# Attention's value product with the values as weights, in high and low halves for nine of sixteen pairs, written straight into the dense stage's input

## The chip, the cores and the metric

The kernel runs on one core of a Trainium2 chip. The metric is the device time of one execution in microseconds (us), of which the median of several runs is quoted. Lower is better.

## What is computed

```python
def _attn_ref(q, k, v, tau):                      # 4 batches, 8 heads, 576 rows, head size 64
    scores = scale * np.matmul(q, k.transpose(0, 1, 3, 2))
    thresh = np.max(scores, axis=-1, keepdims=True) - tau
    scores = np.where(scores >= thresh, scores, -1000000000.0)
    scores = scores - np.max(scores, axis=-1, keepdims=True)
    attn = np.exp(scores)
    attn = attn / (np.sum(attn, axis=-1, keepdims=True) + 1e-09)
    return np.matmul(attn, v)
...
    xk = mu_k * x + (1.0 - mu_k) * x_prev         # first dense stage, x is 4 x 576 x 512
    xr = mu_r * x + (1.0 - mu_r) * x_prev
    k = np.maximum(xk @ w_k, 0.0)
    v = k * k @ w_v
    r = 1.0 / (1.0 + np.exp(-(xr @ w_r)))
    x = r * v
...
    u = x + np.real(np.fft.fft(np.fft.fft(x, axis=1), axis=2))
    un = (u - mean) / np.sqrt(var + 1e-06)        # over the 512 channels
    return u + np.maximum(un @ w_ch1, 0.0) @ w_ch2
```

## The kernel before

**Numbers.** float32 data go through the matrix engine in one of two ways. "Native" is a matmul on float32 operands, which the program emits as two instructions. "In halves" is fp32r: a value is split into a high part (rounded to fp32r) and a low part (the rest), and a product is the sum of fp32r matmuls high x high, low x high and high x low (`three`, lines 706 to 709).

**Work and its order.** Heads are taken in pairs: 16 pairs, four to a batch. A pair has 9 row tiles of 128 queries: tiles 0 to 3 of the first head, tile 4 with the last 64 rows of both heads, tiles 5 to 8 of the second. There are 144 tiles. Every engine runs a loop over slots n (lines 919 to 926 on PE). In slot n:

- PE forms the scores of tile n (`qk`, line 734), transposes the probabilities of tile n-3 (`transpose_probs`, line 747: five blocks of 128 keys), multiplies the transposed probabilities of tile n-4, as weights, with the 64 columns of values (`pv`, line 764, native), and then does its share of the dense work of the batch before.
- DVE takes the row maximum of tile n (`row_max`, line 1235), masks and sums tile n-1 (`mask`, line 1249), and does its share of the dense work.
- ACT forms exp of tile n (line 985), does its share of the dense work, and copies the transposed probabilities of tile n-2 out of PSUM in two pieces (`copy_units`, line 994). At the end of a head `copy_head` (line 1007) copies the head's output into x_att, scaled by the reciprocal row sums.
- POOL splits q and k of the next heads (lines 548 and 556) and forms low halves for the dense stage.
- SP issues the loads.

Each engine works in its own program order. From tile 36 on one PSUM buffer holds scores, so that `qk(n)` waits for `row_max(n-1)`.

**Dense work beside it.** A batch's dense stage runs beside the attention of the next one, at phases counted in slots from the batch's last tile plus one. X_AT (2 to 5): PE transposes x_att (`dense`, lines 839 and 844) and DVE and ACT copy it into xT. MIX_AT (3 to 20): ACT, DVE, ACT and POOL form the mixed inputs mix_v, mix_h and mix_l. Phases 8 to 35: the groups r, k and v, 12 matmuls of 288 columns for a group of r or k and 24 for one of v. FOLD_AT (32, 35): sums on DVE for the Fourier transform. Y_AT (36 to 38) and U_AT (39 to 43): its matmuls, then the additions on POOL (`add_dft`, line 638). So phases 36 to 43 of one batch fall on the first pair of the batch after the next one's start, together with phases 0 to 7 of the next batch. The last batch's dense stage runs alone, and the closing two-layer stage (`mlp`) follows it.

```python
MIX_AT = [3, 4, 5, 6, 7, 8, 9, 10, 12, 13, 14, 15, 17, 18, 19, 20]
U_AT = [39, 39, 42, 42, 43]
...
last = nc.tensor.matmul(bank(6 + p)[:, i * DH:i * DH + width], probsT[:, n % 2, kt * P128:(kt + 1) * P128],
                        v_sb[:, kt, pair % 2, p * DH:p * DH + width], start=kt == 0, stop=kt == KT - 1)
```

## Time and profile before

| | |
|---|---|
| median of 3 runs | 1123.1 us (1122.18 to 1124.58) |
| the profiled execution | 1122.31 us |
| its span in the trace | 1120.5 us |
| PE busy | 1080.2 us, 96% |
| DVE, ACT, POOL busy | 559.9, 515.5, 420.0 us |
| row maxima, first and last start | 9.3 and 578.7 us |

The span is that of the instructions; the rest of the execution lies around it. Busy shares are means over stages with different limits. A matmul's printed duration holds its way through the array, so that matmuls in a row overlap: what one costs is the distance from its start to the next start. The stretches below were cut where the first row maximum of a pair starts: pair 0 starts at 9.3, pair 4 (batch 1) at 93.4, pair 8 at 245.9, pair 12 at 415.5, pair 13 at 459.1, pair 14 at 498.7, pair 15 at 541.7; the last tile's row maximum starts at 578.7.

### The profile page before, as it was taken

The numbers are of one execution on the slowest core, as the hardware profiler recorded it, in microseconds if no ns is written. First come the engines' busy times: TensorE is split into PE (matmuls) and PEld (weight loads), VectorE is DVE, ScalarE is ACT, GpSimd is POOL, SyncE is SP. The second block draws the span as 40 slices with busy tenths as digits, with TensorE's granted clock in tenths as the row PEclk, the third lists the DMA queues.
The fourth block names the chain that finished last, engine by engine and source line by source line (L and its number), as shares of the span: only waits on it lengthen the run. The fifth ranks groups of instructions, "written<-read, shape, count | busy, mean of one in ns | idle before, by whom it ended". The sixth has DMA issues, their size and how long they took to land.

```text
span 1120.5 us, 19690 instructions
## 1 busy us (share of the span) xinstructions
PE 1080.2 (96%) x7476; PEld 1055.1 (94%) x7476; DVE 559.9 (50%) x1109; ACT 515.5 (46%) x1269; POOL 420.0 (37%) x367
## 2 busy tenths in 40 slices
PE   6999999999999999899998998999999999999998
PEld 6899999998899998899996997999999999999998
DVE  7998764576464575564552557453132321323211
ACT  5989775656666646775653733221111111111110
POOL 5897652543662543652512363431111121110100
PEclk9999999999899999999997998999999999999999
DMA  9544101141301141301112107301001010010000
GB/s 244 167 115 151 56 24 34 49 132 35 97 24 34 38 141 36 98 24 34 40 65 94 43 10 281 118 1 57 1 1 57 1 56 0 0 56 0 29 1 29
DMA packets 38353, 69.26 MB, mean 62 GB/s; under 512 B 4214, under 2 KB 19708, under 8 KB 37244
## 3 DMA queue, kind: packets, MB, share of 16 engines
q1 hardware_dynamic: 37964, 67.80, 19.2%
q8 instruction: 53, 0.87, 0.3%
q10 hardware_dynamic: 304, 0.33, 0.1%
q14 instruction: 32, 0.26, 0.1%
HBM read 55.84 MB, written 12.28 MB: 61 GB/s over the span
## 4 chain that ended last, share of the span: by engine, by line
PE 82%; DVE 5%; POOL 5%; issue 3%; ACT 3%; DMA 0%; SPq 0%; DVEq 0%; POOLq 0%; ACTq 0%
PE PB L707 21%; PE PB L709 19%; PE PB L708 19%; PE PB L764 10%; PE PB L734 6%; PE PB L747 5%; DVE probs L1249 1%; POOL mix_l L607 1%; DVE neg_s L1235 1%; POOL q_hl L556 1%; POOL x2T L638 1%; POOL k_lo L548 1%; POOL fold_l L630 1%; ACT exps L985 1%; POOL x2T L639 1%
## 5 line engine op out<-in xcount | busy, mean ns | idle before, releaser
L1187 ACT ACTIVATE h_hi<-PB 128x384 fp32r<-128x384 f32 x96 | 47.2, 492 | 334.7 <-PE PB L709 334.7
L1416 DVE SCALAR_TENSOR_TENSOR h_lo<-PB,h_hi 128x384 fp32r<-128x384 f32 x96 | 53.5, 557 | 260.7 <-ACT h_hi L1187 260.7
L764 PE MATMUL PB<-v_sb,probsT 128*128 128x64 f32 (+1 forms) x1440 | 179.3, 272 | 0.0
L764 PEld LDWEIGHTS PB<-v_sb,probsT 128*128 128x128 f32 x1440 | 174.1, 194 | 0.0
L994 ACT ACTIVATE probsT<-PB 128x384 f32<-128x384 f32 (+1 forms) x288 | 109.3, 432 | 81.6 <-PE PB L747 80.5
L1249 DVE SCALAR_TENSOR_TENSOR probs<-neg_s,thresh,exps 128x576 f32<-128x576 f32 x144 | 145.8, 1012 | 0.0
L1235 DVE TENSOR_SCALAR_CACHE_REDUCE neg_s<-PB,taus 128x576 f32<-128x576 f32 x144 | 117.1, 813 | 40.4 <-PE PB L734 35.8
L707 PE MATMUL PB<-un_h,w1h 128*128 128x384 f32 x384 | 132.3, 345 | 0.0
L709 PE MATMUL PB<-h_hi,w2l 128*128 128x384 f32 x384 | 129.4, 337 | 0.0
L707 PE MATMUL PB<-h_hi,w2h 128*128 128x384 f32 x384 | 129.3, 337 | 0.0
L708 PE MATMUL PB<-un_l,w1h 128*128 128x384 f32 x384 | 129.2, 337 | 0.0
L708 PE MATMUL PB<-h_lo,w2h 128*128 128x384 f32 x384 | 129.2, 336 | 0.0
L709 PE MATMUL PB<-un_h,w1l 128*128 128x384 f32 x384 | 129.1, 336 | 0.0
L985 ACT ACTIVATE exps<-neg_s,negmax 128x576 f32<-128x576 f32 x144 | 111.0, 771 | 0.0
L607 POOL TENSOR_TENSOR mix_l<-mix_v,mix_h 128x288 fp32r<-128x288 f32 x64 | 53.4, 834 | 150.8 <-ACT mix_h L1070 119.9
L747 PE MATMUL PB<-ident,probs 128*128 128x128 f32 x720 | 103.2, 274 | 5.2 <-ACT probsT L994 4.3
L747 PEld LDWEIGHTS PB<-ident,probs 128*128 128x128 f32 x720 | 86.1, 141 | 7.0 <-issue 6.1
L734 PE MATMUL PB<-k_hi,q_hl 128*128 128x288 f32 x320 | 74.7, 315 | 10.0 <-DVE q_hl L1220 7.6
L622 POOL TENSOR_TENSOR k_sql<-k_sq,k_sqh 128x288 fp32r<-128x288 f32 x56 | 48.5, 870 | 90.9 <-DVE k_sq L1331 90.8
L1268 DVE SCALAR_TENSOR_TENSOR mix_v<-xT,mus,mix_v 128x288 f32<-128x288 f32 x64 | 45.7, 713 | 70.8 <-ACT mix_v L1056 70.4
L707 PE MATMUL PB<-mix_h,wkh 128*128 128x288 f32 x256 | 78.8, 308 | 0.9 <-POOL mix_l L607 0.8
L707 PE MATMUL PB<-k_sqh,wvh 128*128 128x288 f32 x256 | 78.7, 307 | 0.1
(154 smaller groups left out, 2485.8 us busy)
## 6 DMA issues: line engine op xcount, KB each, us to landing
q_raw<-qT_dram SPq DMA_DIRECT2D x62, 160.0 KB, 3.1
k_raw<-kT_dram SPq DMA_DIRECT2D x64, 144.0 KB, 3.1
w_raw<-w_dram SPq DMA_DIRECT2D x8, 1024.0 KB, 9.4
cs<-cs_scr SPq DMA_DIRECT2D x4, 1740.0 KB, 7.8
u_scr<-x2T SPq DMA_DIRECT2D x4, 1152.0 KB, 5.2
u_in<-u_scr SPq DMA_DIRECT2D x6, 768.0 KB, 5.0
out_dram<-o_sb SPq DMA_DIRECT2D x24, 192.0 KB, 1.9
cd<-cd_scr SPq DMA_DIRECT2D x4, 1032.0 KB
```

The costliest lines, as they stand in the source:

```text
L607: nc.gpsimd.tensor_tensor(mix_l[kind][:, dt, :], mix_v[:, i % 2, :], mix_h[kind][:, dt, :].bitcast(F32), ALU.subtract).then_inc(mixl_ready, 1)
L707: nc.tensor.matmul(o, ah, rh, start=start, stop=False)
L708: nc.tensor.matmul(o, ah, rl, start=False, stop=False)
L709: return nc.tensor.matmul(o, al, rh, start=False, stop=stop)
L734: last = nc.tensor.matmul(scores(n)[:, half, :], q_hl[:, h, i * P128:(i + 1) * P128], kk[:, h, half * HALF:half * HALF + HALF], start=h == ...
L747: last = nc.tensor.transpose(bank(4 + unit % 2)[:, (kt - k0) * P128:(kt - k0 + 1) * P128], probs[:, n % 2, kt * P128:(kt + 1) * P128], ide ...
L764: last = nc.tensor.matmul(bank(6 + p)[:, i * DH:i * DH + width], probsT[:, n % 2, kt * P128:(kt + 1) * P128], v_sb[:, kt, pair % 2, p * DH ...
L985: nc.scalar.activation(exps[:, n % 2, :], neg_s[:, n % 2, :], ACT.Exp, bias=negmax[:, col:col + 1], scale=-1.0).then_inc(exp_ready, 1)
L994: nc.scalar.activation(probsT[:, n % 2, k0 * P128:k1 * P128], bank(4 + unit % 2)[:, 0:(k1 - k0) * P128], ACT.Copy).then_inc(unit_copied, 1)
L1235: nc.vector.tensor_scalar(neg_s[:, n % 2, :].rearrange("p (a n) -> p a n", a=2), scores(n), taus[:, 2:3], None, ALU.mult, ALU.min, accum_o ...
L1249: nc.vector.scalar_tensor_tensor(probs[:, n % 2, 0:S], neg_s[:, n % 2, :], thresh[:, col:col + 1], exps[:, n % 2, :], ALU.is_le, ALU.mult, ...
L1416: nc.vector.scalar_tensor_tensor(h_lo[:, ft % 3, :], bank(4 + ft % 3)[:, 0:W], 0.0, h_hi[:, ft % 3, :].bitcast(F32), ALU.max, ALU.subtract ...
```

## The change

`native(pair)` is true for the four pairs of batch 0 and for pairs 4, 8 and 12. The other nine are done in halves.

- The value product's operands change places. The values of a pair's two heads (native) are the weights, and the transposed probabilities move through. A pair's product is four chunks of 4 or 5 blocks of 64 queries (256 or 320 columns) over 5 key tiles: 20 matmuls, where 45 stood. In a pair done in halves the weights are one head's [high half, low half] side by side (`vhl`), and the probabilities go through twice, as high and as low half; rows 0 to 63 and 64 to 127 of the output must then be added.
- A tile's transposed probabilities are written to one PSUM tensor and copied by ACT in one instruction (`copy_probs`). For halves the copy is rounded to fp32r, and DVE subtracts it from PSUM for the low half (`lower_probs`). The next tile's transposes wait for both.
- The product comes out as channels x queries, which is the layout of xT. DVE multiplies it with the reciprocal row sums, spread over partitions (inv_rows), and writes xT (`put_out`). For halves ACT first copies one half of the rows out (`copy_half`) and DVE adds the other. `copy_head`, x_att, the transposes of x_att and their copies are gone.
- The reciprocals reach inv_rows by way of DRAM: SP stores them for each head, element by element, waits for the landing, and loads them to 64 partitions (`spread_inverse`).
- exp is written into probs, of which there are three buffers, and masked in place. Halves of v: ACT `v_high`, POOL `v_low`, for nine pairs. q and k have one raw buffer after batch 0. xT and the fold buffers are double. MIX_AT's last entries are a slot later, U_AT becomes 39, 39, 40, 40, 41. k_sq is squared in place after ACT's square.

```diff
+    return pair < PAIRS or pair % PAIRS == 0                      # native(pair)
+CHUNK_END = [1, TAIL, 6, 8]
+CHUNK_BLOCKS = [(1, 5), (0, 5), (1, 5), (1, 6)]
+PV_AT = {True: {6: [(0, 0, 2)], 7: [(0, 2, 4)], 8: [(0, 4, 5)], 9: [(1, 0, 2)], 10: [(1, 2, 5)],
+                11: [(2, 0, 3)], 12: [(2, 3, 5)], 13: [(3, 0, 2)], 14: [(3, 2, 5)]},
+         False: {5: [(0, 0, 5)], 8: [(1, 0, 5)], 10: [(2, 0, 5)], 12: [(3, 0, 5)]}}
+OUT_AT = {True: {9: 0, 10: 1, 12: 2, 14: 3}, False: {7: 0, 9: 1, 12: 2, 13: 3}}
+VHL_AT = (1, 5)
...
+                def spread_inverse(head):
+                    sp.wait_ge(inv_ready, head + 1)
+                    sp.dma_start(inv_scr[pair, tiles, :].rearrange("t p -> p t"), rowinv[:, tiles], allow_slow_non_contiguous=True).then_inc(inv_out, 16)
+                    sp.wait_ge(inv_out, 16 * head + 16)
+                    if pair > 0:
+                        sp.wait_ge(x_out, 4 * (pair - 1) + 2 + 2 * p)
+                    flat = inv_scr[pair, :, :].rearrange("t p -> (t p)")
+                    if p == 0:
+                        sp.dma_start(inv_rows[0:DH, :], flat[0:S].partition_broadcast(DH)).then_inc(inv_in[0], 16)
...
-                    for unit, k0, k1 in units_of(n):
-                        if unit >= 2:
-                            pe.wait_ge(unit_copied, unit - 1)
+                    if n > 0:
+                        pe.wait_ge(pT_copied, n)
+                        if not native((n - 1) // TILES_PAIR):
+                            pe.wait_ge(pT_lowered, lows_before(n))
+                    for kt in range(KT):
+                        last = nc.tensor.transpose(PB[2][:, kt * P128:(kt + 1) * P128], probs[:, n % 3, kt * P128:(kt + 1) * P128], ident[:, :])
+                    last.then_inc(pT_ready, 1)
...
+                        for kt in range(k0, k1):
+                            nc.tensor.matmul(o, vhl[h][:, kt, :], pT_hi[:, kt, b0:b1, :], start=kt == 0, stop=False)
+                            last = nc.tensor.matmul(o, vhl[h][:, kt, :], pT_lo[:, kt, b0:b1, :], start=False, stop=kt == KT - 1)
...
-                    for dt in range(DT):
-                        yield X_AT[dt]
-                        pe.wait_ge(head_out, d * H + 2 * dt + 2)
-                        for st in range(FULL):
-                            last = nc.tensor.transpose(ring(d, "x", 0, dt)[:, st * P128:(st + 1) * P128], x_att[:, st, dt * P128:(dt + 1) * P128], ident[:, :])
...
+                def lower_probs(n):
+                    dve.wait_ge(pT_copied, n + 1)
+                    nc.vector.tensor_tensor(blocks_of(pT_lo, jj), transposed(), blocks_of(pT_hi, jj).bitcast(F32), ALU.subtract).then_inc(pT_lowered, 1)
+                def put_out(pair, chunk):
+                    if native(pair):
+                        dve.wait_ge(pv_done, index + 1)
+                        src = bank(6 + chunk % 2)
+                    else:
+                        dve.wait_ge(half_copied, order + 1)
+                        nc.vector.tensor_tensor(half_sum[rows, 0:n], bank(6 + chunk % 2)[rows, 0:n], half_sum[rows, 0:n], ALU.add).then_inc(half_summed, 1)
+                        dve.wait_ge(half_summed, order + 1)
+                        src = half_sum
+                    if chunk % 2 == 0:
+                        dve.wait_ge(inv_in[chunk // 2], (16, 32)[chunk // 2] * (pair + 1))
+                    nc.vector.tensor_tensor(xT[b % 2][rows, dt, 1 + first:1 + last], src[rows, skip:n], inv_rows[rows, first:last], ALU.mult).then_inc(x_out, 1)
```

PE's order in the slot of tile 59 (the sixth tile of pair 6), from the scores to the first dense matmul, before:

```order
L734 MATMUL PB<-k_lo,q_hl 128x288 x2
L747 MATMUL PB<-ident,probs 128x128 [waits unit_copied,probs_ready]
L747 MATMUL PB<-ident,probs 128x128 x2
L747 MATMUL PB<-ident,probs 128x128 [waits unit_copied]
L747 MATMUL PB<-ident,probs 128x128
L764 MATMUL PB<-v_sb,probsT 128x64 [waits unit_copied]
L764 MATMUL PB<-v_sb,probsT 128x64 x4
L707 MATMUL PB<-mix_h_83,wrh 128x288 [waits r_out]
```

The end of the same slot's value product in the change (chunk 0 of pair 6, its last four of ten matmuls), and what follows it:

```order
L894 MATMUL PB<-pT_hi,vhl_73 128x256
L895 MATMUL PB<-pT_lo,vhl_73 128x256
L894 MATMUL PB<-pT_hi,vhl_73 128x256
L895 MATMUL PB<-pT_lo,vhl_73 128x256
L870 MATMUL PB<-ident,probs 128x128 [waits pT_lowered,pT_copied,probs_ready]
L870 MATMUL PB<-ident,probs 128x128 x4
L829 MATMUL PB<-mix_h_103,wrh 128x288 [waits r_out]
```

The product now stands ahead of the transposes, in four of a pair's nine slots, and the transposes wait for DVE's subtraction too.

DVE's order in the slot of tile 52 (the eighth tile of pair 5), before:

```order
L1235 TENSOR_SCALAR neg_s,negmax<-PB,taus 128x576 [waits probs_ready,scores_ready]
L1249 SCALAR_TENSOR_TENSOR probs,rowsum<-neg_s,thresh,exps 128x576 [waits unit_ready,thr_ready,exp_ready]
L1331 TENSOR_TENSOR k_sq<-k_relu 128x288 [waits k_out]
L1235 TENSOR_SCALAR neg_s,negmax<-PB,taus 128x576 [waits probs_ready,scores_ready]
L1249 SCALAR_TENSOR_TENSOR probs,rowsum<-neg_s,thresh,exps 128x576 [waits unit_ready,thr_ready,exp_ready]
```

The same slot in the change:

```order
L1352 TENSOR_SCALAR neg_s,negmax<-PB,taus 128x576 [waits probs_ready,scores_ready]
L1360 SCALAR_TENSOR_TENSOR probs,rowsum<-neg_s,thresh,probs 128x576 [waits thr_ready,exp_ready]
L1377 TENSOR_TENSOR pT_lo<-PB,pT_hi 128x5x2x64 [waits pT_copied]
L1396 TENSOR_TENSOR half_sum<-PB,half_sum 64x256 [waits half_copied]
L1407 TENSOR_TENSOR xT_92<-half_sum,inv_rows 64x256 [waits inv_in0,half_summed]
L1414 SCALAR_TENSOR_TENSOR mix_raw_105<-xT_85,mus,mix_raw_105 128x288 [waits mixt_r]
L1465 TENSOR_TENSOR k_sq<-k_sq 128x288 [waits ksqh_ready]
```

Between the mask and the dense work stand the subtraction for the low half and the two steps of `put_out`; the mixing step comes from the slot after.

SP's order for one pair of batch 1 in the change (heads' loads, the reciprocals of a pair's first head, the values, the next head):

```order
L484 DMA k_main<-kT_dram 64x576
L514 DMA inv_scr<-rowinv 128x5x1 [waits inv_ready]
L521 DMA inv_rows<-inv_scr 64x576 [waits x_out,inv_out]
L506 DMA v_raw<-v_dram 128x4x128 [waits v_split]
L507 DMA v_raw<-v_dram 64x128
L483 DMA q_main<-qT_dram 64x640 [waits qk_split]
L484 DMA k_main<-kT_dram 64x576
```

The values' load and the next head's load are queued behind the landing of the reciprocals' store.

## Rows read from the trace of the kernel before

**Rows 1.** Windows: length, busy us (PE, PEld, DVE, ACT, POOL), clock, DMA share, GB/s.

```profile
9.30:93.40 84.10, 78.31 (x648) 75.94 (x648) 79.82 (x160) 73.97 (x189) 72.86 (x50) 1.00 0.65 195
...
245.90:415.50 169.60, 165.57 (x1289) 161.50 (x1288) 99.36 (x229) 106.70 (x282) 79.93 (x77) 0.98 0.20 61
415.50:459.10 43.60, 39.56 (x298) 35.50 (x298) 25.61 (x61) 27.25 (x73) 23.54 (x24) 1.00 0.24 70
459.10:498.70 39.60, 39.48 (x317) 39.25 (x316) 25.94 (x57) 31.06 (x83) 24.52 (x24) 1.00 0.21 67
498.70:541.70 43.00, 43.00 (x348) 43.00 (x347) 21.32 (x51) 26.35 (x69) 15.09 (x14) 1.00 0.08 23
...
578.70:618.80 40.10, 34.37 (x193) 29.51 (x192) 14.20 (x33) 15.70 (x44) 11.73 (x14) 0.74 0.32 111
...
719.00:1120.50 401.50, 396.96 (x2253) 393.86 (x2252) 113.61 (x162) 64.67 (x109) 54.60 (x34) 1.00 0.06 22
```

**Rows 2.** The page: the chain that ended last, by engine.

```profile
PE 82%; DVE 5%; POOL 5%; issue 3%; ACT 3%; DMA 0%; SPq 0%; DVEq 0%; POOLq 0%; ACTq 0%
```

**Rows 3.** Timeline of PE in one slot: start, us, line, operation, count.

```profile
301.39 0.43 PE L734 MATMUL PB<-k_hi,q_hl 128*128 128x288 f32 x2
301.66 0.43 PE L734 MATMUL PB<-k_lo,q_hl 128*128 128x288 f32 x2
301.92 0.71 PE L747 MATMUL PB<-ident,probs 128*128 128x128 f32 x5
302.47 1.23 PE L764 MATMUL PB<-v_sb,probsT 128*128 128x64 f32 x10
303.50 0.38 PE L707 MATMUL PB<-mix_h,wkh 128*128 128x288 f32 x1
303.72 0.29 PE L708 MATMUL PB<-mix_l,wkh 128*128 128x288 f32 x1
```

**Rows 4.** Timeline of PE, Fourier and closing stages.

```profile
697.61 0.28 PE L708 MATMUL PB<-cd,fold_h 128*128 128x258 f32 x1
697.73 0.28 PE L709 MATMUL PB<-cd,fold_l 128*128 128x258 f32 x1
...
718.81 0.34 PE L709 MATMUL PB<-h_hi,w2l 128*128 128x384 f32 x1
718.99 0.81 PE L773 MATMUL PB<-part,mean 128*128 128x384 f32 x2
719.34 0.63 PE L707 MATMUL PB<-un_h,w1h 128*128 128x384 f32 x1
719.81 0.34 PE L708 MATMUL PB<-un_l,w1h 128*128 128x384 f32 x1
```

**Rows 5.** Groups by form: count, busy us, mean ns, idle before.

```profile
L1249 DVE SCALAR_TENSOR_TENSOR probs<-neg_s,thresh,exps 128x576 f32<-128x576 f32 x144 | 145.8, 1012 | 0.0
L1105 ACT ACTIVATE k_sqh<-k_relu 128x288 fp32r<-128x288 f32 x64 | 28.5, 445 | 2.0
L1442 DVE TENSOR_TENSOR o_sb<-PB,u_in 128x384 f32<-128x384 f32 x24 | 11.7, 549 | 31.3 <-PE PB L709 31.3
L839 PE MATMUL PB<-ident,x_att 128*128 128x128 f32 x64 | 10.4, 290 | 5.4 <-ACT x_att L1007 3.2 <-DVE summ L1379 1.4 <-DVE y_l L1372 0.7
L1388 DVE TENSOR_TENSOR pair_sum<-x2T 128x576 f32<-128x576 f32 x8 | 6.0, 748 | 0.1
```

**Rows 6.** Timeline of PE at phase 8 of batches 1 and 2.

```profile
286.34 0.40 PE L707 MATMUL PB<-mix_h,wrh 128*128 128x288 f32 x1 [2.71 <-POOL mix_l L607]
...
456.01 0.40 PE L707 MATMUL PB<-mix_h,wrh 128*128 128x288 f32 x1 [2.72 <-POOL mix_l L607]
```

**Rows 7.** Windows: the stretch after the first of them.

```profile
287.70:294.50 6.80, 6.80 (x32) 6.78 (x31) 3.46 (x9) 4.83 (x12) 3.44 (x5) 0.50 0.45 173
```

**Rows 8.** DMA issues: count, KB each, median us from issue to landing.

```profile
k_raw<-kT_dram SPq DMA_DIRECT2D x64, 144.0 KB, 3.1
...
taus<-tau_dram ACTq DMA_DIRECT2D x1, 0.5 KB, 4.4
```

More of the change, by code:

```diff
@@ L128, in bank_turns @@
     for i, group in enumerate(order):
-        if alone(group[0]) and group[1] != "x":
+        if alone(group[0]):
             of[group] = (6, 5, 0, 1, 2, 3)[several % 6]
@@ L680, in _ @@
                     pair, jj = n // TILES_PAIR, n % TILES_PAIR
-                    for step in second_head.get(jj, ()):
+                    for step in (early_second if pair < PAIRS else second_head).get(jj, ()):
                         split_step(pair, 1, step)
@@ L686, in _ @@
                     setup_at(n)
+                    for h in range(2):
+                        if jj == VHL_AT[h] + 1 and not native(pair):
+                            v_low(pair, h)
                     run_beside(beside, n)
@@ L921, in _ @@
                         qk(n)
+                    for pair, at in pairs_near(n):
+                        for chunk, k0, k1 in pv_parts(pair).get(at, ()):
+                            pv(pair, chunk, k0, k1)
                     if 0 <= n - 3 < TILES:
                         transpose_probs(n - 3)
-                    if 0 <= n - 4 < TILES:
-                        pv(n - 4)
                     run_beside(beside, n)
@@ L1017, in weight_hi, with v_high @@
+                def v_high(pair, h):
+                    act.wait_ge(v_in[pair % 2], 32 * (pair // 2) + 32)
+                    act.wait_ge(pv_done, 4 * pair if h else 4 * pair - 2)
+                    nc.scalar.activation(vhl[h][:, :, 0:DH], v_raw[:, :, h * DH:(h + 1) * DH], ACT.Copy).then_inc(vh_ready, 1)
                 def weight_hi(n):
@@ L1173, in _ @@
                     weight_hi(n)
+                    for pair, at in pairs_near(n):
+                        if not native(pair) and at in VHL_AT:
+                            v_high(pair, VHL_AT.index(at))
+                        if not native(pair) and at in OUT_AT[False]:
+                            copy_half(pair, OUT_AT[False][at])
                     run_beside(beside, n)
                     if 0 <= n - 2 < TILES:
-                        copy_units(n - 2)
-                    if 0 <= n - 5 < TILES and (n - 5) % TILES_PAIR in (TAIL, TILES_PAIR - 1):
-                        copy_head(n - 5)
+                        copy_probs(n - 2)
                 def chunk(c, p, first, more):
@@ L1406, in _ @@
                         mask(n - 1)
+                    if 0 <= n - 3 < TILES and not native((n - 3) // TILES_PAIR):
+                        lower_probs(n - 3)
+                    for pair, at in pairs_near(n):
+                        if at == 4 and native(pair) and pair > PAIRS:
+                            dve.wait_ge(pv_done, 4 * pair)
+                            nc.vector.memset(v_place(pair)[64:128, KT - 1, :], 0.0).then_inc(v_padded, 1)
+                        if at in OUT_AT[native(pair)]:
+                            put_out(pair, OUT_AT[native(pair)][at])
                     if n == WEIGHTS_FROM:
```

434 lines of the change are left out of this document (243 added, 191 removed).

## Prediction

> **What bounds the kernel now.** I read the chain of the page first: PE holds 82% of it, every other engine 5% or less [rows 2]. Then I cut the span into stretches, since the change touches the time to 618.8 only; the last batch's dense stage stays, and so does the closing stage, 401.5 us of it in the last row [rows 1]. Three regimes are to be seen there.
>
> In batch 0 (9.3 to 93.4) no dense stage runs beside the attention. PE is busy 78.3 of 84.1 us, DVE 79.8, ACT 74.0, POOL 72.9. All engines are nearly full, DVE the fullest: what DVE gains there costs time.
>
> In the batches with a dense stage beside them PE is the bound: in the pairs from 459.1 and 498.7 it is busy 39.5 of 39.6 and 43.0 of 43.0 us, with DVE at 25.9 and 21.3. The first pair of a batch (415.5 to 459.1) has 4 us in which PE stands: 39.6 of 43.6.
>
> After the last row maximum (578.7 to 618.8) PE is busy 34.4 of 40.1 us, and its mean clock is 0.74: a mixture of its two levels, 2.4 and 1.2 GHz. There is time in waits and at the low level.
>
> **The value product on PE.** A tile now takes ten instructions from 302.47 to 303.50, 1.03 us [rows 3], a pair 9 x 1.03 = 9.27. Their number sets this, not their columns.
>
> In halves a pair takes 20 instructions of 256 columns and 20 of 320. The nearest rows: 258 columns step by 0.12 us (697.61 to 697.73), 288 by 0.13 (two from 301.39 to 301.66), 384 by 0.18 (718.81 to 718.99) [rows 3, 4]. So 0.12 and 0.147: 20 x 0.12 + 20 x 0.147 = 5.3 us. Nine pairs save 9 x (9.27 - 5.3) = **35.6 us**.
>
> Native, the two instructions of a 384-column matmul hold PE from 718.99 to 719.81 less one step of 0.17, so 0.65 us, 1.7 ns a column [rows 4]. 256 and 320 columns take 0.43 and 0.54, a pair 10 x 0.43 + 10 x 0.54 = 9.7. Seven pairs lose 7 x 0.43 = **3 us**.
>
> Could the fp32r steps be shorter than linear? The rows say that 384 columns take 0.17 to 0.18, so the step follows the columns. The Trainium skill ("TensorE: Matmul & The Clock Gate", Back-to-back issue gap) gives a sustained 81 ns a matmul at 128 columns and 131 ns at 512. By an estimate between those figures 256 and 320 columns would take 98 and 106 ns and a pair 4.1 us, and the nine pairs would save 11 us more. The rows disagree with it, 0.17 us at 384 columns, and I go by them.
>
> **The transposes of x_att** disappear: 16 of 128 columns and 4 small ones a batch at 0.11 (five in 0.55 us [rows 3]), 2.2 us, so 8.8 in all, and 5.4 us of idle time stood before the large ones [rows 5]. Those waits are for copies and banks, some of which have successors in the new chain. I take **12 us** of the 14.
>
> **The first pair of a batch.** At phase 8 the group r waits 2.7 us for mix_l on POOL, behind `add_dft` [rows 6]; it occurs twice, and after the first time the clock is 0.50 for 6.8 us, which costs 3.4 [rows 7]. The change puts `add_dft` two slots earlier, so the 8.8 us may vanish. But POOL also has q and k to split there. I take **5**. After the attention, mean clock 0.74 over 40 us is some 10 us of lost clock; fewer waits should give part of it back: **3**, between nothing and 8.
>
> Gains: 35.6 - 3 + 12 + 5 + 3 = 52.6 us.
>
> **What DVE gets.** `lower_probs`, 81 times 640 columns from PSUM: 384 take 549 ns, 576 from SBUF 748 [rows 5], so 0.82 us, 66 us. `put_out`: native about 1.7 us a pair (four products, 0.38 us for 256 columns by the same slope, and a short one), in halves 0.75 a chunk, 3 a pair. ACT loses `copy_head` and has one copy for two; it is not near the bound.
>
> In batch 0 four pairs bring 4 x 1.7 = 6.8 us to the fullest engine. I count **7**, and **2** for waits for inv_rows (below).
>
> In a pair in halves DVE gets 9 x 0.82 + 3 = 10.4 us. Then the pair from 498.7 has 31.7 of DVE beside 43 - 4 = 39 of PE, which is enough room. The fourth pair of a batch: the batch from 245.9 has 99.4 us of DVE in 169.6; less the three pairs that stand singly (72.9 in 126.2) that leaves 26.5 in 43.4, of which 3.4 are the low clock. So 26.5 + 10.4 = 36.9 of DVE beside 40 - 4 = 36 of PE: full. The second pair (from 459.1) saves PE nothing, as native chunks of the pair before run into it, and has 33.5 beside 39.5. On the mean DVE about fits under PE, and the coupling is now tighter: the transposes of tile n-3 wait for DVE's subtraction of tile n-4, one slot old, where they waited for a copy on ACT. In a slot with k groups DVE also waits for ACT's square (0.45 us [rows 5]) and not only its relu, and the Fourier sums (two of 0.75 us and small ones [rows 5], twice a batch) stand in one lump ahead of the next subtraction. A lump or a late k_sq pushes the subtraction past the point where PE wants it. I charge 2 us for each of the six third and fourth pairs and 1 for each second: **15 us**. Bounds: nothing, if a slot's slack takes it; 35, the whole saving.
>
> What is queued behind DVE's waits is the next row maximum, for which PE's scores wait.
>
> Sum: -52.6 + 7 + 2 + 15 = -29 us. Span 1120.5 - 29 = 1091.5. The profiled run took 1122.3, 1.8 above its span, and the median is 1123.1: **1093 us**.
>
> **The reciprocals through DRAM** cost nothing in this sum because slots cover them. A store and a load lie between DVE's reciprocal and its `put_out`. Rows: a load of 144 KB lands after 3.1 us, 128 elements of 4 bytes after 4.4 at the start [rows 8]. Round trip some 7 us. Halves: from slot 5 to slot 7, two slots of 4.3, 8.6 us. Batch 0: four and three slots of 2.3, 9.2 and 6.9, hence the 2 us above. No row shows 640 separate elements going out; lower bound 3.1 + 1.9 or so (nothing waits), upper open.
>
> **Rivals.**
>
> *The saving arrives whole.* PE never waits for DVE and the first pairs lose their stalls: 35.6 - 3 + 14 + 8.8 + 8 = 63, less 7 in batch 0, 56 us: 1067. For it: DVE at 50 to 65% in those pairs. Against: in batch 0, where two engines are nearly full, PE still stands 6 us of 84. Chance 0.18.
>
> *DVE becomes the bound.* The third and fourth pairs give back nothing (26 us lost rather than 12), the second pairs get 3 us longer (9, not 3): 20 us above the forecast, 1113. For it: the in-order engine has waits on three others in each slot, and the mask, which reads two SBUF tensors of 576, takes 1.01 us on the mean where a sum of two such tensors takes 0.75 [rows 5]. Chance 0.16.
>
> *Slower: the reciprocals come late.* If the round trip takes T, a pair in halves waits T - 8.6 in `put_out` (9 times), a native pair of batch 0 T - 9.2 and T - 6.9 (4 times each). With T = 12 that is 31 + 11 + 20 = 62 us less the 2 counted, and PE's idle stretches bring the low clock besides: 1153. It decides from about T = 10 (13 + 3 + 12 = 28). For it: stores of 4 bytes, 512 or 640 to a head, an SP queue that waits for each landing, and DMA engines 65% busy in batch 0. Against: 128 such elements landed in 4.4 us. Chance 0.12. The Trainium skill ("DMA: Bandwidth & Descriptors", Specifications and Anatomy of one DMA) speaks for it: below 512 bytes a transfer does a read-modify-write, and a DMA's fixed cost of about 2 us is mostly the receipt from the target memory, longest for DRAM. By its fixed cost alone, an estimate, two legs would take 4 us and nothing would wait; what 640 rewrites add it does not say.
>
> *Nothing moves* (within 0.2%, about what a measurement of this kernel can tell from no change): a blend of the last two. Chance 0.03.
>
> The forecast itself, 1078 to 1108, has 0.51. Faster 0.84, same 0.03, slower 0.13. The range leaves out the slower case and the very end of the clean one: 1062 to 1121.
>
> **What would show it.** Step by step: value instructions in halves start 0.12 and 0.147 us apart, native ones 0.21 and 0.27; no idle time of 2.7 us at phase 8; DVE busy near 560 + 66 + 33 = 655 us; batch 0 some 9 us longer; first pairs near 36 us, third pairs near 40; PE's waits in the third and fourth pairs end with the subtraction. Wrong would be: DVE idle before the multiplication by inv_rows (the rival on T), or PE's pairs as long as before with DVE over 90% busy.

## The result, and the profile after

The change makes the kernel slower: 1179.58 us (median of 4 runs, 1177.53 to 1182.99) against 1122.64 us for the kernel before on the same chip, a ratio of 1.0507 with a 95% interval of 1.0478 to 1.0536. The forecast was 1093. The rival that I had given 0.12, the reciprocals that come late, is what happened. Its price was 1153.

Windows of the changed kernel, cut at the first row maximum of a pair as in [rows 1]: batch 0, the first pair of batch 1, then pairs 12 to 14 (length, busy us of PE, PEld, DVE, ACT, POOL, clock, DMA share, GB/s).

```profile
9.20:128.00 118.80, 85.83 (x456) 71.32 (x457) 75.45 (x173) 67.00 (x127) 66.94 (x47) 0.88 0.42 109
128.00:172.40 44.40, 28.56 (x150) 22.97 (x150) 23.87 (x51) 20.36 (x42) 21.21 (x19) 0.86 0.42 112
...
473.20:512.40 39.20, 32.38 (x205) 28.57 (x206) 31.59 (x68) 24.39 (x55) 23.86 (x23) 0.93 0.24 68
512.40:557.80 45.40, 43.29 (x293) 40.57 (x293) 32.10 (x69) 29.12 (x66) 25.27 (x26) 0.96 0.33 83
557.80:601.40 43.60, 40.48 (x307) 39.33 (x306) 33.24 (x70) 26.83 (x58) 16.79 (x17) 1.00 0.20 44
```

Batch 0 took 84.1 us and takes 118.8; no engine is full there any more. The first pair of batch 1 took 29.2 and takes 44.4. These two stretches hold 50 of the 61 us by which the span grew (1120.5 to 1181.2). Their clock was 1.00 and is 0.88 and 0.86, so that by an estimate up to 14 and 6 us of their lengths are the low clock's (12% and 14%). From there on the pairs are about as long as they were: 39.2, 45.4 and 43.6 us where [rows 1] has 43.6, 39.6 and 43.0.

The chain that ended last, by engine and then the start of it by line (the page), answers to [rows 2]:

```profile
PE 58%; DMA 16%; DVE 9%; POOL 6%; issue 5%; SPq 3%; ACT 3%; DVEq 0%; ACTq 0%; POOLq 0%
PE PB L829 17%; PE PB L831 16%; PE PB L830 16%; DMA inv_scr<-rowinv 11%; DMA inv_rows<-inv_scr 3%; PE PB L856 3%; DVE probs L1360 2%; PE PB L870 2%; PE PB L887 2%; DVE neg_s L1352 2%; PE PB L894 1%; PE PB L895 1%; POOL mix_l L723 1%; POOL q_hl L667 1%; DVE pT_lo L1377 1%
```

PE fell from 82 to 58%, and DMA, nothing before, has 16%: the store of the reciprocals alone 11%. The waits of DVE, POOL and SP's queue in the changed kernel (waiting instruction, what ended the wait, us in total, times, longest):

```profile
DVE xT L1407 <- DMA inv_rows<-inv_scr: 92.2, 19, 12.7
```

```profile
POOL k_hi L644 <- DMA k_main<-kT_dram: 83.5, 10, 19.0
```

```profile
SPq L521 <- DMA inv_scr<-rowinv: 137.3, 16, 10.7
SPq L523 <- DMA inv_scr<-rowinv: 126.8, 15, 12.6
```

SP waits 264 us in 31 waits for the landing of a store of 2.5 or 2 KB, 8.5 us each. One head of pair 7 in full, first on SP's queue and then on DVE (start, us, line, operation, idle before):

```profile
241.41 0.37 SPq L514 DMA_DIRECT2D inv_scr<-rowinv  x1
251.51 0.45 SPq L521 DMA_DIRECT2D inv_rows<-inv_scr  x1
```

```profile
241.20 0.19 DVE L1372 RECIPROCAL rowinv<-rowinv 128x5 f32<-128x5 f32 x1
...
254.70 0.42 DVE L1407 TENSOR_TENSOR xT<-half_sum,inv_rows 64x256 f32<-64x256 f32 x1 [4.55 <-DMA inv_rows<-inv_scr]
```

From the reciprocal at 241.2 to its use at 254.7 it is 13.5 us: 10.1 for the landing of the store, 3.2 for the load. My T was 7. DVE stands 4.55 us in `put_out`, and behind it wait the next row maximum and PE's scores.

### The profile page after: what moved, and what is told of

Same layout as the page of the kernel before. It is cut to its first block, busy times and chain, and to the rows that moved or that the text cites. A ratio compares the mean times of both kernels' runs of the same rounds, so it can differ in the third digit from the quotient of the medians.

```text
span 1181.2 us, 17994 instructions
## 1 busy us (share of the span) xinstructions
PE 1058.3 (90%) x6596; PEld 999.7 (85%) x6596; DVE 652.1 (55%) x1299; ACT 489.0 (41%) x1011; POOL 430.4 (36%) x385
## 4 chain that ended last, share of the span: by engine, by line
PE 58%; DMA 16%; DVE 9%; POOL 6%; issue 5%; SPq 3%; ACT 3%; DVEq 0%; ACTq 0%; POOLq 0%
PE PB L829 17%; PE PB L831 16%; PE PB L830 16%; DMA inv_scr<-rowinv 11%; DMA inv_rows<-inv_scr 3%; PE PB L856 3%; DVE probs L1360 2%; PE PB L870 2%; PE PB L887 2%; DVE neg_s L1352 2%; PE PB L894 1%; PE PB L895 1%; POOL mix_l L723 1%; POOL q_hl L667 1%; DVE pT_lo L1377 1%
## 5 line engine op out<-in xcount | busy, mean ns | idle before, releaser
L1360 DVE SCALAR_TENSOR_TENSOR probs<-neg_s,thresh,probs 128x576 f32<-128x576 f32 x144 | 149.1, 1035 | 0.4 <-ACT probs L1100 0.2
L856 PE MATMUL PB<-k_hi,q_hl 128*128 128x288 f32 x320 | 78.6, 328 | 52.6 <-DVE neg_s L1352 32.2
L870 PE MATMUL PB<-ident,probs 128*128 128x128 f32 x720 | 108.4, 284 | 17.0 <-DVE pT_lo L1377 13.1
L870 PEld LDWEIGHTS PB<-ident,probs 128*128 128x128 f32 x720 | 89.3, 147 | 33.5 <-DVE probs L1360 13.4
L1100 ACT ACTIVATE probs<-neg_s,negmax 128x576 f32<-128x576 f32 x144 | 110.1, 764 | 0.0
L856 PEld LDWEIGHTS PB<-k_hi,q_hl 128*128 128x128 f32 x320 | 52.8, 200 | 60.3 <-DVE neg_s L1352 24.1
L1116 ACT ACTIVATE pT_hi<-PB 128x640 fp32r<-128x640 f32 x81 | 56.9, 703 | 106.0 <-PE PB L870 106.0
L887 PE MATMUL PB<-pT_native,v_native 128*128 128x256 f32 (+1 forms) x280 | 85.8, 441 | 16.7 <-DVE xT L1407 16.7
L723 POOL TENSOR_TENSOR mix_l<-mix_raw,mix_h 128x288 fp32r<-128x288 f32 x64 | 54.5, 855 | 97.1 <-ACT mix_h L1184 95.4
L887 PEld LDWEIGHTS PB<-pT_native,v_native 128*128 128x128 f32 x280 | 54.5, 208 | 27.9 <-issue 18.1
```

The costliest lines, as they stand in the source:

```text
L723: nc.gpsimd.tensor_tensor(mix_l[kind][:, dt, :], mix_raw[kind][:, dt, :], mix_h[kind][:, dt, :].bitcast(F32), ALU.subtract).then_inc(mixl_ ...
L856: last = nc.tensor.matmul(scores(n)[:, half, :], q_hl[:, h, i * P128:(i + 1) * P128], kk[:, h, half * HALF:half * HALF + HALF], start=h == ...
L870: last = nc.tensor.transpose(PB[2][:, kt * P128:(kt + 1) * P128], probs[:, n % 3, kt * P128:(kt + 1) * P128], ident[:, :])
L887: last = nc.tensor.matmul(o, v_place(pair)[:, kt, :], pT_native[chunk % 2][:, kt, b0:b1, :], start=kt == 0, stop=kt == KT - 1)
L1100: nc.scalar.activation(probs[:, n % 3, 0:S], neg_s[:, n % 2, :], ACT.Exp, bias=negmax[:, col:col + 1], scale=-1.0).then_inc(exp_ready, 1)
L1116: nc.scalar.activation(blocks_of(to, jj), transposed(), ACT.Copy).then_inc(pT_copied, 1)
```

## The experiments

Each run is compared with the kernel before on its own chip, which took 1124.4 us for the first four runs of the table, 1123.4 for the next four, 1123.8 for low_twice to rows_act, 1122.7 for store_sizes and rows_actq, 1123.2 for rows_act7 and 1122.7 for rows_both.

| run | us | ratio (95%) |
|---|---|---|
| no_recip | 1118.60 | 0.9947 (0.9922 to 0.9971) |
| store_20b | 1124.81 | 1.0012 (0.9987 to 1.0036) |
| late_load | 1182.50 | 1.0512 (1.0460 to 1.0564) |
| rows_512b | 1124.96 | 1.0014 (0.9988 to 1.0039) |
| no_low | 1102.86 | 0.9808 (0.9754 to 0.9862) |
| old_u_at | 1121.99 | 0.9979 (0.9950 to 1.0007) |
| rows_sp | 1124.17 | 1.0004 (0.9979 to 1.0030) |
| all_native | 1166.46 | 1.0372 (1.0314 to 1.0429) |
| low_twice | 1135.60 | 1.0109 (1.0075 to 1.0142) |
| cols_1234 | 1163.60 | 1.0349 (1.0314 to 1.0383) |
| rows_pool | 1123.57 | 0.9999 (0.9981 to 1.0016) |
| rows_act | 1122.82 | 0.9991 (0.9975 to 1.0008) |
| store_sizes | 1127.79 (one run) | |
| rows_actq | 1123.36 | 0.9996 (0.9975 to 1.0017) |
| rows_act7 | 1126.26 | 1.0033 (1.0016 to 1.0050) |
| rows_both | 1123.93 | 0.9994 (0.9970 to 1.0019) |

**Is it the reciprocals' way?** no_recip takes it out:

```diff
                 def spread_inverse(head):
+                    return
...
+                nc.gpsimd.memset(inv_rows[:, :], 0.01)
...
-                            dve.wait_ge(inv_out, 16 * (head - 1))
...
-                        dve.wait_ge(inv_in[chunk // 2], (16, 32)[chunk // 2] * (pair + 1))
```

> The changed kernel without the way of the reciprocals through DRAM: the store, the wait for its landing and the loads are gone, and inv_rows holds a constant (the normalisation by the row sums is left out). All else stays: the subtraction in every pair in halves, put_out, the place of add_dft. Theory A (the reciprocals' way is the whole of the miss): DVE's 92 us of waits for inv_rows and POOL's 84 us for k_main go, batch 0 takes about 90 us, and the time is 1080 to 1100 us, near my forecast of 1093. Theory B (DVE's subtractions and their coupling with PE hold the pairs, and the waits for inv_rows only stand where other waits would): 1140 us or more. In between, 1105 to 1135, both have a part.

It took 1118.6 us, 61 less than the changed kernel, and fell between the two theories: the reciprocals make the kernel slower than before, but they are not the whole of the miss. Its windows (batch 0, the first pair of batch 1, then the first three pairs of batch 3):

```profile
9.10:96.80 87.70, 77.08 (x458) 63.70 (x459) 83.60 (x173) 66.22 (x127) 70.94 (x50) 1.00 0.61 180
```

```profile
96.80:126.30 29.50, 24.62 (x150) 20.45 (x149) 24.69 (x51) 20.13 (x42) 21.14 (x17) 1.00 0.21 54
...
414.20:453.10 38.90, 32.09 (x205) 28.07 (x206) 31.53 (x69) 24.37 (x55) 23.84 (x23) 0.96 0.35 116
453.10:498.80 45.70, 43.43 (x292) 40.17 (x291) 34.18 (x69) 29.09 (x66) 25.29 (x25) 0.96 0.15 44
498.80:539.90 41.10, 39.45 (x302) 38.70 (x302) 34.51 (x71) 26.55 (x58) 17.95 (x18) 1.00 0.13 39
```

Batch 0 is back at 87.7 us and the pair behind it at 29.5.

**What makes the store slow?** store_20b writes the same bytes as 128 runs of 20 or 16 bytes; late_load moves the wait for the landing behind the other loads in SP's order; rows_512b has PE transpose the reciprocals and stores five rows of 512 bytes:

```diff
# store_20b
-sp.dma_start(inv_scr[pair, tiles, :].rearrange("t p -> p t"), rowinv[:, tiles], allow_slow_non_contiguous=True)
+sp.dma_start(inv_scr[pair, tiles, :].rearrange("t p -> (t p)").rearrange("(p t) -> p t", p=P128), rowinv[:, tiles])
# late_load: the lines of spread_inverse from the wait for inv_out on become load_inverse
+                    if jj == 1 and pair > 0:
+                        load_inverse(2 * pair - 1)
...
+                    if jj == 7:
+                        load_inverse(2 * pair)
# rows_512b
+                        last = nc.tensor.transpose(PB[2][0:QT - head % 2, KT * P128:(KT + 1) * P128],
+                                                   rowinv[:, QT:TILES_PAIR] if head % 2 else rowinv[:, 0:QT], ident[:, :])
...
+                        nc.scalar.activation(rowT[0:QT - head % 2, head % 2, :], PB[2][0:QT - head % 2, KT * P128:(KT + 1) * P128], ACT.Copy).then_inc(invT_copied, 1)
...
+                    sp.dma_start(inv_scr[pair, tiles, :], rowT[0:QT - p, p, :]).then_inc(inv_out, 16)
```

> The changed kernel with one edit: the store of a head's reciprocals writes 128 runs of 20 (16) bytes instead of 640 (512) single elements of 4 bytes, same bytes, same waits (the reciprocals land in another order, so the normalisation uses wrong rows; nothing else is touched). If the number of separate elements sets the time to the landing (some 9 us now), it should fall to about 4 us, as for the 128 elements of 4 bytes at the start (4.4), and the kernel to 1100 to 1130 us. If the landing has a floor of its own, or the queue or the busy DMA engines make it, the landing stays at 8 us or more and the kernel within 10 us of 1180.

> The changed kernel with the wait for the landing and the load moved one or two slots behind the store in SP's order, so that the loads of q, k and v that stood behind that wait are issued before it. Theory A1 (a large part of the loss is the next heads' k and q coming late, POOL's 84 us of waits for k_main, because SP stands in the wait for the landing): batch 0 gets 10 to 25 us shorter, the time falls to 1150 to 1170 us. Theory A2 (only the way from the reciprocal to put_out counts): the waits of DVE for inv_rows stay or grow a little, the time is 1178 to 1195 us.

> The changed kernel, complete, with another way for the reciprocals: PE transposes rowinv (five columns) behind the five transposes of the tile before, ACT copies the result to SBUF, and SP stores five (four) rows of 512 bytes; loads as before. It adds 24 small transposes and 24 small copies, some 0.3 us each on engines with room, and about 1 us to the chain. If the number of elements sets the landing: store some 3 us, way from reciprocal to put_out some 8 us, and the time 1095 to 1120 us. If the landing has a floor of 8 us whatever is stored: 1180 to 1195 us.

store_20b took 1124.8 and rows_512b 1125.0 us: what store_20b alone changes is worth 55 us of the 61. SP's waits for the landing in store_20b:

```profile
SPq L523 <- DMA inv_scr<-rowinv: 30.7, 16, 4.7
...
SPq L521 <- DMA inv_scr<-rowinv: 21.5, 16, 4.0
```

52 us in 32 waits where there were 264, and POOL's waits for k_main fell from 83.5 to 31.9 us. late_load took 1182.5: with the other loads issued first the kernel gains nothing (A2 held), though POOL's wait for k_main fell from 83.5 to 59.5 us. So their place behind SP's wait is not the main cause. The edit also moves the reciprocals' load a slot or two later, which can hide a small gain.

I took the number of elements for the reason. cols_1234 stores 128, 256, 384 and 512 of them in turn (and loads only 128), and store_sizes other lengths and distances (its loads read another tensor):

```diff
# cols_1234
+                    cols = slice(tiles.start, tiles.start + head % 4 + 1)
+                    sp.dma_start(inv_scr[pair, cols, :].rearrange("t p -> p t"), rowinv[:, cols], allow_slow_non_contiguous=True)
# store_sizes
+                    to, n = ((flat[0:256], 2), (flat[SQ:SQ + 512], 1), (flat[0:SQ], 4), (flat[SQ:SQ + 512], 3))[head % 4]
+                    sp.dma_start(to.rearrange("(p t) -> p t", p=P128)[:, 0:n], rowinv[:, tiles.start:tiles.start + n], allow_slow_non_contiguous=True)
```

> The changed kernel, with the store of head h cut to the first h mod 4 + 1 of its columns: 128, 256, 384 and 512 single elements of 4 bytes in turn, and a load of 128 elements to 64 partitions for each head (left out: the other reciprocals, so most of the output has a wrong scale). If the landing follows the number of elements, SP waits some 2, 4, 6 and 8 us for the four sizes, first heads (128 and 384 elements) half as long as the 8.6 us they take now, and the kernel lands between 1119 and 1180, about 1135. If single elements of 4 bytes have a floor whatever their number, all four wait 8 us and the time is 1170 or more.

> The changed kernel with four forms of the store in turn over the heads, 128 runs each: 8 bytes side by side (heads 0, 4, ...), single 4 bytes with 16 bytes from one to the next (heads 1, 5, ...), 16 bytes with 20 from one to the next (heads 2, ...), 12 bytes with 16 from one to the next (heads 3, ...). The loads read 64 rows of another tensor, so the reciprocals are not used (the normalisation is left out). If only the size of a run of 4 bytes makes the landing long: the second form takes 7 us, the first, third and fourth 1.4 to 2 us. If it is neighbours that lie side by side within a few bytes: the first takes 7 us, the second 1.4 to 2. If every run under 16 bytes is slow: first, second and fourth 7 us, third 1.4.

SP's queue in cols_1234, a store of 128 elements and the load that waits for it, then one of 512:

```profile
317.21 0.34 SPq L515 DMA_DIRECT2D inv_scr<-rowinv  x1
323.71 0.45 SPq L524 DMA_DIRECT2D inv_rows<-inv_scr  x1
...
377.62 0.37 SPq L515 DMA_DIRECT2D inv_scr<-rowinv  x1
385.40 0.46 SPq L526 DMA_DIRECT2D inv_rows<-inv_scr  x1
```

After batch 0 the stores of 128 elements took 6.5 to 7.6 us to the next issue, those of 512 7.0 to 8.3. A quarter of the elements takes off one microsecond: the number is not it, and my expectation fell. SP's queue in store_sizes, heads 12 to 14 (8 bytes side by side, single 4 bytes every 16, 16 bytes every 20):

```profile
198.64 0.33 SPq L516 DMA_DIRECT2D inv_scr<-rowinv  x1
201.32 0.47 SPq L523 DMA_DIRECT2D inv_rows<-ident_dram  x1
215.97 0.33 SPq L516 DMA_DIRECT2D inv_scr<-rowinv  x1
217.79 0.47 SPq L523 DMA_DIRECT2D inv_rows<-ident_dram  x1
237.57 0.33 SPq L516 DMA_DIRECT2D inv_scr<-rowinv  x1
238.97 0.47 SPq L523 DMA_DIRECT2D inv_rows<-ident_dram  x1
```

2.7, 1.8 and 1.4 us from the store's issue to the next. The 12-byte form took 1.4 to 4.8 us. Its longest, of heads 7, 15 and 23 (4.5 to 4.8), say little on the form, since with runs of 20 or 16 bytes the same three heads took 4.2 to 5.1 us, two of them right behind the load of the table cs (1740 KB). Head 15 in store_20b:

```profile
255.55 1.73 SPq L538 DMA_DIRECT2D cs<-cs_scr  x1
259.21 0.33 SPq L514 DMA_DIRECT2D inv_scr<-rowinv  x1
264.32 0.46 SPq L523 DMA_DIRECT2D inv_rows<-inv_scr  x1
```

Single elements of 4 bytes are quick (1.4 to 2.4 us after batch 0) when they lie 16 bytes apart and slow (7 us) when they lie side by side; 8 bytes side by side take 2.7 to 3.1. So neither the number nor the size of the elements alone sets the time. How many of them share a small stretch of DRAM would fit all the forms; it was not varied by itself, and what the memory does with them the trace does not show.

**Where the other 25 us are.** no_low leaves DVE's subtraction and PE's waits for it out, low_twice makes it nearly twice, old_u_at puts the Fourier groups and the last mixing steps back; all three stand on no_recip:

```diff
# no_low
-                        lower_probs(n - 3)
...
-                            last = nc.tensor.matmul(o, vhl[h][:, kt, :], pT_lo[:, kt, b0:b1, :], start=False, stop=kt == KT - 1)
+                            last = nc.tensor.matmul(o, vhl[h][:, kt, :], pT_hi[:, kt, b0:b1, :], start=False, stop=kt == KT - 1)
# low_twice
+                    nc.vector.tensor_tensor(spare[:, :, :, :], transposed()[:, 0:4], blocks_of(pT_hi, jj)[:, 0:4].bitcast(F32), ALU.subtract)
# old_u_at
-MIX_AT = [3, 4, 5, 6, 7, 8, 9, 10, 13, 14, 15, 16, 18, 19, 20, 21]
+MIX_AT = [3, 4, 5, 6, 7, 8, 9, 10, 12, 13, 14, 15, 17, 18, 19, 20]
-U_AT = [39, 39, 40, 40, 41]
+U_AT = [39, 39, 42, 42, 43]
```

> The kernel without the reciprocals' way (1118.6 us) and also without DVE's 81 subtractions for the low halves; PE runs the same number of instructions, with the high half of the probabilities twice (left out: the low halves of the probabilities, and the normalisation). Theory C (the 25 us that are still missing are PE's waits for a DVE that is too full in the pairs in halves: 14.5 us for the row maximum, 13.3 for the subtraction): they go, DVE gets 66 us less, and the time is 1090 to 1099 us. Rival (PE's own work makes the second pairs long, the native product of the pair before running into them, and the waits only stand where others would, for ACT's copies): 1108 us or more.

> The kernel without the reciprocals' way (1118.6 us; the normalisation is left out) with more work for DVE instead of less: before each subtraction it makes another one over 512 of the 640 columns into a spare tile that nobody reads, 81 times some 0.67 us, 54 us in all. Taking 66 us away gave 15.8. Theory C (in the third and fourth pairs of a batch DVE, busy 84 and 92%, is at its bound, in the others it has room): a pair gets 6 us of DVE, the fourth pairs give nearly all of it back as time, the third half, the second a third: +25 to +35 us, 1144 to 1154. Rival (PE's waits come from the order in which DVE's work stands and not from its amount, so the idle time takes it): +12 or less, under 1131.

> The kernel without the reciprocals' way (1118.6 us), with U_AT and MIX_AT of the kernel before (last Fourier groups and their sums on POOL two slots later, the last mixing steps one slot earlier). My prediction gave 5 us to the earlier place of the sums. If that holds, this takes 1122 to 1125 us. If the move is worth nothing, since POOL is late for mix_l at either place (10.9 us of PE's waits are left), 1117 to 1120. If the earlier place makes new waits (3 us each for mid_l and fold_l stand in the trace), 1112 to 1116.

no_low took 1102.9 us, 15.8 less than no_recip, and low_twice 1135.6, 17.0 more, by the intervals of the ratios give or take some 7 and 5 us. Both effects were smaller than theory C had it and larger than the rival's. Windows of the second, third and fourth pair of batch 2, of no_low and of low_twice:

```profile
282.40:326.10 43.70, 41.85 (x293) 39.12 (x292) 30.50 (x63) 29.01 (x66) 24.93 (x25) 1.00 0.15 43
326.10:365.20 39.10, 39.10 (x306) 39.09 (x305) 28.52 (x60) 26.90 (x58) 18.06 (x18) 1.00 0.14 41
365.20:402.60 37.40, 35.08 (x268) 34.19 (x266) 28.03 (x72) 20.30 (x44) 19.54 (x18) 1.00 0.18 56
```

```profile
295.40:343.10 47.70, 44.74 (x294) 41.35 (x294) 36.84 (x76) 28.81 (x66) 25.68 (x26) 0.94 0.14 40
343.10:386.00 42.90, 39.67 (x302) 38.63 (x301) 38.38 (x79) 26.58 (x58) 16.46 (x16) 1.00 0.14 37
386.00:427.30 41.30, 36.81 (x272) 34.77 (x270) 39.39 (x90) 20.74 (x45) 19.96 (x18) 1.00 0.20 60
```

Around no_recip (45.5, 40.7 and 39.4 us) each pair moves by about 2 us either way, in the pairs where DVE is at 76% as in those at 92%. A microsecond of these instructions costs 0.24 us (15.8 of 66) to 0.31 (17 of 55): DVE is no full bound in these pairs, and it is not free in them. Counted by DVE's busy time the second figure is 0.52, since that rose by 32.5 us only (677.3 to 709.8): other instructions came out shorter, k_sq 533 ns on the mean where it took 626.

old_u_at took 1122.0, 3.4 more. That is near the 5 us of my sum but not clear of noise, the intervals of the two ratios overlap. Its windows say more: the first pair of batch 3 and the stretch behind the last row maximum in old_u_at, then that stretch in no_recip:

```profile
418.50:465.10 46.60, 35.92 (x207) 31.13 (x208) 29.63 (x68) 24.27 (x55) 22.55 (x23) 0.85 0.33 106
583.90:1120.00 536.10, 517.40 (x3028) 505.35 (x3026) 192.67 (x286) 123.50 (x235) 112.29 (x91) 0.98 0.13 47
```

```profile
573.80:1117.50 543.70, 522.53 (x3028) 509.16 (x3026) 192.51 (x286) 123.57 (x235) 112.92 (x91) 0.96 0.13 46
```

At their old places the sums make the first pairs of batches 2 and 3 47.0 and 46.6 us long, at a clock of 0.85, where no_recip has 38.8 and 38.9 at 0.96: the earlier place (with the later mixing steps) is worth 8 us in each. It costs 0.4 to 1.6 us in each second and third pair, and behind the last row maximum no_recip is 7.6 us longer, with 4.2 us of PE's waits for mix_l against 0.8. How much of the 7.6 is the edit's stays open: in the traces of the other runs, all with the new places, this stretch takes 537 to 544 us.

all_native, on rows_sp, has `native` return True:

> As rows_sp, but with the value product in native form in all 16 pairs: the change of operands alone, without halves. PE gets nine times 10.5 us of value product where it has 5.4 (+46 us); DVE loses 81 subtractions and half of put_out (about 85 us), and with them PE's waits for it (up to 28). Theory C (waits for DVE are real and go with its work): 1118 + 46 - 25 = about 1139 us, 1132 to 1146. Rival (the waits are others' and stay): 1160 us or more.

It took 1166.5 us, 42 more than rows_sp. In no_recip five native matmuls of 256 columns take 2.16 us (462.54 to 464.70) and five of 320 2.69 (467.37 to 470.06), so a native pair is 9.7 us, as in my prediction and not the 10.5 of this expectation, and nine pairs bring PE 40 us. They arrive whole, and DVE's busy time, 75 us less (596.4 against 671.2), gives nothing back. The rival held. PE waits for POOL more instead (12.4 us for q_hl and 13.1 for mix_l from 90 to 640 us, against 4.3 and 8.3). So the price of DVE's work found above holds for the kernel it was measured in. The halves are the part of the change that pays, 4.7 us a pair for nine pairs.

**Can it be had?** With quick stores the complete kernel equals the kernel before. Left over against no_recip are 8 us in the first pair of batch 1 (37.4 us in rows_512b, 29.5 without the reciprocals). Six kernels went after them, all with rows of 512 bytes: rows_sp has SP store the dense tables in slot 36 and not 34, rows_pool has POOL do it in slot 32, rows_act ACT in slot 34; rows_actq gives the reciprocals to ACT's queue, rows_act7 only those of heads 7 to 31, rows_both is that with the tables on POOL.

```diff
# rows_sp
-                    if n == 34:
+                    if n == 36:
                         sp.wait_ge(odd_rounded, 1)
# rows_pool (rows_act: act and nc.scalar, n == 34)
+                    if n == 32:
+                        pool.wait_ge(odd_rounded, 1)
+                        pool.wait_ge(tables_split, 5)
+                        nc.gpsimd.dma_start(cd_scr[:, 0], cd_hi[:, :, :].bitcast(F32)).then_inc(tables_stored, 16)
...
# rows_actq, in copy_probs on ACT (rows_act7: only for head >= 7)
+                        nc.scalar.dma_start(inv_scr[pair, tiles, :], rowT[0:QT - head % 2, head % 2, :]).then_inc(inv_out, 16)
+                    if jj in (TAIL, TILES_PAIR - 1):
+                        load_inverse(2 * pair + half_of(n))
```

> The complete kernel with the reciprocals stored as rows of 512 bytes (1125.0 us), and in SP's order the store of the five dense tables, for whose halves it waits, put behind the store of head 7's reciprocals instead of ahead of it. If that wait is what makes the first pair of batch 1 take 37.4 us where it takes 29.5 without the reciprocals, the time falls by 6 to 8 us to 1117 to 1119, that is 0.5% below the kernel before. If something else holds that pair (q late at POOL), it stays at 1123 to 1126.

> The complete kernel with the reciprocals as rows of 512 bytes (1125.0 us), and the five stores of the dense tables issued by POOL in slot 32 in place of SP in slot 34. The first pair of batch 1 takes 37.4 us, where it takes 29.5 without the reciprocals: on SP the wait for the tables' halves stands ahead of the store for head 7, and behind it ACT's mixing waits for the tables (6.2 us). If both waits go with this, 1117 to 1119 us, 0.5% below the kernel before. If POOL, full in batch 0, comes later with the tables: 1123 to 1130.

> As rows_pool, but the five stores of the tables are issued by ACT in its slot 34, which waits there for POOL's last half. ACT has some 15% of room in batch 0. If the order on SP was the cause of the long first pair of batch 1: 1117 to 1120 us. If ACT stands long for POOL's last table, or the issues themselves (five, about a microsecond each) are what counts: 1122 to 1127.

> The complete kernel with the reciprocals as rows of 512 bytes (1125.0 us), with their stores and loads issued by ACT: the store in the slot of the copy, the load a slot later, when the store has landed. SP no longer waits for a reciprocal or a landing. ACT gets some 2.3 us of issuing a pair. If SP's order is what is left of the loss: the first pair of batch 1 takes 30 to 31 us, where it took 37.4, and the kernel 1118 to 1121 us, 0.3 to 0.5% below the kernel before. If ACT, 85% busy in batch 0, becomes late by its new work, or the first pair stays at 35 or more: 1123 us or more.

> The complete kernel with the reciprocals as rows of 512 bytes; heads 0 to 6 are stored and loaded by SP (as in rows_512b, 1125.0 us), heads 7 to 31 by ACT (as in rows_actq, 1123.4 us). If the two losses are apart in place (ACT late in the first pair of batch 0, SP late ahead of batch 1), both go: batch 0 as in rows_512b, the first pair of batch 1 about 30 us, the kernel 1117 to 1120 us, 0.3 to 0.6% below the kernel before. If batch 0 ends later by what the first pair of batch 1 gains, 1122 to 1125.

> rows_act7 (1126.3 us) with the five stores of the dense tables issued by POOL in slot 32, as in rows_pool. If the load of k_main beside the tables' stores is what holds the first pair of batch 1 (12.7 us of POOL's waits), that wait falls under 4 us, the pair from 39 to about 31, and the kernel to 1117 to 1120 us. If the load collides with the tables at whatever place, since both are wanted in the same 10 us at the end of batch 0, the pair stays at 35 or more and the kernel at 1122 to 1126.

None is below the kernel before by more than the measurement's width; rows_act7 is 0.3% above it. In rows_actq the first pair of batch 1 takes 29.7 us as hoped, but the first pair of batch 0, where DMA is busy at 94%, grew to 21.7 (windows, then ACT's waits there):

```profile
9.10:30.80 21.70, 15.31 (x87) 12.68 (x88) 16.13 (x37) 12.04 (x25) 14.55 (x12) 0.99 0.94 269
101.30:131.00 29.70, 24.62 (x149) 20.41 (x150) 24.09 (x52) 21.36 (x47) 21.17 (x17) 1.00 0.22 63
```

```profile
ACT thresh L1086 <- DMA inv_scr<-rowT: 4.4, 1, 4.4
```

In rows_act7 that first pair is short again, but the pair behind batch 0 takes 39.1 us, and POOL waits there for k, loaded beside SP's stores of the tables:

```profile
POOL k_hi L649 <- DMA k_main<-kT_dram: 12.7, 1, 12.7
```

rows_both brings the pair to 32.6, and the pair behind it is 1.3 us longer. The loss moves from one wait to the next; which order would be free of it stays open.

## Why the prediction was wrong

**The step that failed** is "the reciprocals through DRAM cost nothing in this sum because slots cover them", with T at some 7 us. Measured: 12.7 to 22.7 us from a reciprocal to its use for the eight heads of batch 0 and 13.5 in the head shown; SP waits 8.5 us on the mean for a store's landing. The row that I held against the rival was of the wrong kind: the 4.4 us of [rows 8] are those of a load, and nothing in the trace of before showed a store of single elements. The prediction said so, called the upper end open, and still let the range stop at 1121. The rival's sum for T = 12 was 62 us, 31 of them in batch 0; measured between the changed kernel and no_recip are 61, and 31 in batch 0 (118.8 to 87.7). The sum hit by luck in part: T was longer, slots that are already late cover more of it, and k for the next heads, which comes late behind SP's waits, was not in it. The Trainium skill ("DMA: Bandwidth & Descriptors", Specifications) says that below 512 bytes a transfer does a read-modify-write. It gives no time for it, and by the size alone the runs here can't be ordered: single 4 bytes that lie 16 bytes apart land in 1.8 us, side by side in 7. That neighbours wait for each other's rewriting would fit both, but no run here shows it.

**The second miss, 23 to 26 us** (forecast -29, no_recip -6 by its median, -3 by its span), term by term:

- The value product in halves was right. Timeline of PE in the changed kernel, to set beside [rows 3]:

```profile
381.56 0.31 PE L895 MATMUL PB<-pT_lo,vhl 128*128 128x320 f32 x1
381.71 0.31 PE L894 MATMUL PB<-pT_hi,vhl 128*128 128x320 f32 x1
...
391.45 0.28 PE L895 MATMUL PB<-pT_lo,vhl 128*128 128x256 f32 x1
391.57 0.28 PE L894 MATMUL PB<-pT_hi,vhl 128*128 128x256 f32 x1
```

  0.12 us for 256 columns and 0.145 for 320, the steps of the sum. The native steps were right too (0.43 and 0.54 us a matmul). The third pairs came out at 40.7 to 41.1 us (forecast 40), the fourth 1.3 to 3.1 shorter than before.
- Batch 0: +3.6 us in no_recip, where the sum had +7 without the 2 for inv_rows. The pair behind it gains nothing (29.5 us, it was 29.2).
- DVE's 15 us: 15.8 measured by no_low, give or take 7. Right in size. I had put 12 of the 15 into the third and fourth pairs; measured are 1.7 to 2.0 us in each of these but the last (0.5), and 1.0 to 1.8 in the second pairs too. `lower_probs` is 65.8 us (66 in the sum), and DVE was busy 652.1 us in the changed kernel (655).
- The first two pairs of a batch are the term that was mis-sized. I had 36 us for the first and 1 us more for the second. The second pairs of no_recip are 3.9, 3.1 and 6.1 us longer than before, the first pairs of batches 2 and 3 only 4.7 shorter. In batch 3 the two take 38.9 and 45.7, together 84.6 us, where [rows 1] has 83.2. PE's waits in the first of them without the reciprocals:

```profile
PE PB L831 <- POOL mix_l L725: 3.6, 1, 3.6
PE PB L858 <- DVE neg_s L1354: 2.1, 2, 1.2
PE PB L831 <- POOL fold_l L748: 1.6, 1, 1.6
```

  The wait for mix_l of [rows 6] has not gone: it is 3.6 us here and 2.6 in batch 2, where it was 2.7, and two for the row maximum are new. The clock falls to 0.50 twice, at the start of the first pair and behind the wait for mix_l:

```profile
416.00:419.00 3.00, 3.00 (x14) 2.82 (x14) 2.93 (x5) 1.36 (x4) 3.00 (x4) 0.50 0.94 380
453.50:456.50 3.00, 3.00 (x11) 2.33 (x10) 1.82 (x8) 0.45 (x1) 0.00 (x0) 0.50 0.37 103
```

  Before, it was 1.00 in both pairs. The waits of the two pairs are 9.5 us against 3.9, and the low clock costs by an estimate 3.4 us (4% of 84.6) against nothing: 9 us, which took all that the shorter value product and the missing transposes of x_att gave in these pairs. In batch 2, where the kernel before has its own low clock [rows 7], the two pairs are 1.6 us shorter than before. The native product of the first pair also stands mostly in the second (30 of its 40 instructions, windows of that line alone):

```profile
414.20:453.10 38.90, 2.87 (x11) 2.03 (x12) 0.96 0.35 116
453.10:498.80 45.70, 8.79 (x30) 5.42 (x28) 0.96 0.15 44
```

- The stretch behind the last row maximum: 3 us of gain forecast, 1.9 us of loss measured (541.8 to 543.7 us). old_u_at, with the old places, took 536.1 us there. So the change of places that I counted as a gain pays in the first pairs and may be what costs here; one profiled execution of each, beside the scatter named above, does not settle it. What else makes POOL late in these stretches stays open.
